# Weight loads cut into quarters, a moved product and moved softmax weights in a fused attention and MoE kernel

## The chip, the cores and the metric

One core of one Trainium2 chip. The metric is device time in microseconds (us) of one execution. Engine names are those of the profile: PE (matmul) with PEld (its weight load), DVE, ACT, POOL, SP. SP issues the large loads and does nothing else; its DMAs go to the queue called q1, hardware_dynamic. DMAs that POOL issues go to q0, software_dynamic. Both queues are served by the same 16 DMA engines.

## The reference, cut to what matters

```python
# 1. decayed linear attention over q, k, v -> x  [3072 tokens, 512]
logits = x @ phi                                   # 2. soft MoE: 8 experts, 4 slots each
d = exp(logits - logits.max(0)); d /= d.sum(0) + 1e-9
slot_input = (d.T @ x).reshape(8, 4, 512)
slot_out[e] = maximum(slot_input[e] @ w1a[e], 0) @ w2a[e]
c = exp(logits - logits.max(1)); c /= c.sum(1) + 1e-9
x2 = c @ slot_out
noisy = x2 @ w_gate + log1p(exp(x2 @ w_noise)) * noise     # 3. top-2 MoE
top2 = the two largest of noisy; top2_w = exp(top2_l - max) / (sum + 1e-9)
for e, k: out[mask] += top2_w * (maximum(x2[mask] @ w1b[e], 0) @ w2b[e])
```

w1a, w2a (moe_w1, moe_w2) are the weights of the soft MoE, w1b, w2b (moe2_w1, moe2_w2) those of the top-2 MoE. Each has 8 units, one for each expert, of 2,048 KB (2.097 MB): 128 partitions with 16 KB each.

## The kernel before

The work has four stages on one core.

- **Attention and logits** (to about 140 us): 24 tiles of 128 tokens, with chunk loads and halves of w1a on SP's queue.
- **Slots** (to about 183 us): PE multiplies the slot inputs by w1a (L794) and w2a (L814), expert after expert. `ring_used` counts the units that PE has used up; SP's later loads wait for it, since they land in the same places.
- **Passage** (183 to about 250 us): it has two strands. The *choice* strand: gate logits (L838), softplus and choice of the two experts (DVE L1404 to L1420), counts by two matmuls with a triangle and with ones (L885, L886), positions (L1424 to L1449), then a record for each (token, choice) pair (c row in two halves, weight, destinations: 35 words) which POOL writes to DRAM in one DMA of 840 KB (L560, 128 partition rows of 6,720 bytes). A sort by matmuls (L875) gives `idx`, and POOL fetches records in the new order, 128 at a time, by an indirect DMA (L574). The *SW* strand: since x2 = c @ slot_out, the kernel forms SW[e] = slot_out @ w1b[e] for each expert (`sw_product(e)`, L850; a unit of w1b by one product), takes its largest magnitude (ACT `sw_sums`, L1061), scales it and splits it into two f16 parts (`sw_high` on ACT L1065, `sw_low` on DVE L1471), spreads these over the partitions with two matmul groups for each expert (`sw_spread_parts`, L863: a "unit" is a half of an expert), and copies them back (`sw_keep`: ACT L1071 for units 0 to 7 and 12 to 15, DVE L1478 for 8 to 11).
- **Tiles** (from about 246 us): for each of 55 tiles of 128 sorted records `stage_c`, `turn_c` (L903), `hidden_b` (L922), `h_high` and `h_low`, `out_b` (L939), then POOL writes or adds rows to the output.

All order is written out by hand, by engine; each engine runs its list in order and waits on semaphores. Around the change the lists are:

- SP: w2a[2..7] (`load_w2a`), w2b[0], w1b[0..7] (`load_w1b`, L486), w2b[1] (`load_w2b`, L466, after `order_ready`), w2b[2], ... w1b[6] waits for product 2, w1b[7] for product 3 (`ring_used` 2E+3 and 2E+4).
- PE: products 0 to 4, sort (three parts, L875), product 5, product 6, spreads 0 to 3, `turn_c(0)` (needs record tile 0, staged by ACT), product 7, `hidden_b(0)`, first part of `out_b(0)`, spreads 4 to 7, `hidden_b(1)`, and the loop. A spread waits for the copy of the unit three before it, as the three banks are used in turn.
- ACT: sums of w2b[0], `sw_sums(0)`, `w2b_high(0)`, `sw_sums(1)`, Exp of the gap (L1090), `sw_sums` 2, 3, one of the sort's inputs (L1095), `sw_sums(4)`, `sw_high` 0 to 3, `sw_sums` 5, 6, keeps 0 to 3, `stage_c(0)` (L1107), keeps 4 to 7, `keep_ct(0)`, `stage_c(1)`, `sw_sums(7)`, `h_high(0)`, ..., `sw_high` 4 to 7, sums of w2b[1] (L1049), keeps 12 to 15, `h_high(1)`.
- DVE: choice, `w2b_scale_by_sum(0)`, wait for the counts, positions, destinations (L1456), the two weights of each token (L1459 to L1462), digits and comparison tables for the sort (L1495 to L1500), `idx`, `sw_low` 0 to 3, ...
- POOL: record write (L560), largest of SW[0..3], then the fetches, with the largest of SW[4..7] after the sixth.

`w2b[1]` is `w2b_in[EARLY]` in the code, since EARLY is 1; REP is 4, E is 8.

Of the kernel before, what the change touches and what calls it, by code (L numbers as in the profile page):

```python
# [9 lines left out]
ALU = mybir.AluOpType  # L10
# [5 lines left out]
def build_program(nc, chunks, phi, w1a, w2a, w_gate, w_noise, noise, w1b, w2b, consts, out, dims):  # L16
# [40 lines left out]
    with ExitStack() as ctx:  # L57
# [3 lines left out]
        def sem(name):  # L61
            return ctx.enter_context(nc.semaphore(name))
# [215 lines left out]
        w1a_last_full = sem("w1a_last_full")  # L278
        w2a_full = [sem(f"w2a_full{e}") for e in range(E)]
        w1b_full = [sem(f"w1b_full{e}") for e in range(E)]  # L280
        ring_used = sem("ring_used")
        w2b_full = [sem(f"w2b_full{e}") for e in range(E)]
        w2b_sum_ready = sem("w2b_sum_ready")
# [76 lines left out]

        SW_GROUPS = ((0, 4), (4, E))
        W2B_SUMS = 2
        sw_out = [ps[:, 2 + e // 2, e % 2 * QF:(e % 2 + 1) * QF] for e in range(E)]
        SC = ((0, 1), (2, 3))
        Y, ST, T_X, LG = range(4, 8)
# [37 lines left out]
        @block.sync  # L403
        def _(sp):
            def load_words(to, g, at, full):
                sp.dma_start(to.unsqueeze(1), chunks[bass.ds(g, 1), :, at:at + to.shape[1]]
                             .rearrange("g p m -> p g m")).then_inc(full, 16)

            def load_kv(g):
                if g >= KV_DEPTH:  # L410

                    sp.wait_ge(scores_ready, g - KV_DEPTH + 1)
                    sp.wait_ge(v_decayed, g - KV_DEPTH + 1)
                load_words(kv_in[g % KV_DEPTH], g, 0, kv_full[g % KV_DEPTH])

            def load_qk(g):
                if g >= QK_DEPTH:
                    wait_consumed(sp, (g - QK_DEPTH) // NC, (g - QK_DEPTH) % NC)
                load_words(qk_in[g % QK_DEPTH], g, 2 * DM, qk_full[g % QK_DEPTH])

            load_words(kv_in[0][:, 0:DM], 0, 0, turned_full)
            load_words(qk_in[0][:, 0:DM], 0, 2 * DM, turned_full)
            sp.dma_start(const_sb[:, 0:y_dec_at], consts[:, 0:y_dec_at]).then_inc(const_full, 16)
            load_words(kv_in[0][:, DM:2 * DM], 0, DM, kv_full[0])
            load_words(qk_in[0][:, DM:2 * DM], 0, 3 * DM, qk_full[0])
            load_kv(1)
            load_qk(1)
            sp.dma_start(const_sb[:, y_dec_at:ident_at], consts[:, y_dec_at:ident_at]).then_inc(y_dec_full, 16)
            load_qk(2)
            load_kv(2)  # L430
            sp.dma_start(phi_sb[:, :, :], phi.rearrange("(c p) s -> p c s", p=P)).then_inc(phi_full, 16)
            sp.dma_start(ident_stack[:, :], consts[:, ident_at:ident_at + P + SL]).then_inc(ident_full, 16)

            HALF = UNIT // 2

            def w1a_half(e, half, full):
                words = slice(half * HALF, (half + 1) * HALF)
                sp.dma_start(w1a_home[e][:, words], w1a[e, :, words]).then_inc(full, 16)

            ahead = 0  # L440
            for g in range(3, NT):
                load_qk(g)
                load_kv(g)
                more = (g - 2) * 2 * (E - 1) // (NT - 3)
                for half in range(ahead, more):
                    w1a_half(half // 2, half % 2, w1a_early)
                ahead = more
                if g == NC:
                    sp.dma_start(gates[:, :, 0:E], w_gate.rearrange("(c p) e -> p c e", p=P)).then_inc(small_full, 16)
                    sp.dma_start(gates[:, :, E:2 * E], w_noise.rearrange("(c p) e -> p c e", p=P)).then_inc(small_full, 16)  # L450
            assert ahead == 2 * (E - 1)

            def load_w2b(o):

                if o in (3, 6):

                    sp.wait_ge(w2b_lo_ready, {3: 2, 6: 1}[o])
                else:
                    sp.wait_ge(ring_used, {1: E + 3, 2: 2 * E + 6, 4: 2 * E + 7, 5: 2 * E + 8, 7: 2 * E + 2}[o])
                if o == EARLY:  # L460
                    sp.wait_ge(order_ready, 1)
                else:

                    sp.wait_ge(h_hi_ready, 3 * (o - EARLY) - 2)
                e = sp.value_load(order_expert[0:1, o:o + 1], min_val=0, max_val=E - 1)
                sp.dma_start(w2b_in[o].unsqueeze(1), w2b[bass.ds(e, 1), :, :]  # L466
                             .rearrange("e p m -> p e m")).then_inc(w2b_full[o], 16)

            def load_first_w2b():

                sp.wait_ge(ring_used, E + 2)
                sp.dma_start(w2b_in[0], w2b[0, :, :]).then_inc(w2b_full[0], 16)

            def load_w2a_words(e, first, last):
                words = slice(first, last)
                sp.dma_start(w2a_home[e][:, words], w2a[e, :, words]).then_inc(w2a_full[e], 16)

            def load_w2a(e):

                sp.wait_ge(ring_used, (None, None, 1, 2, 3, 5, 7, 8)[e])  # L480
                sp.dma_start(w2a_home[e], w2a[e, :, :]).then_inc(w2a_full[e], 16)

            def load_w1b(e):

                sp.wait_ge(ring_used, (E + 1, E + 6, E + 4, E + 5, E + 7, E + 8, 2 * E + 3, 2 * E + 4)[e])
                sp.dma_start(w1b_home[e], w1b[e, :, :]).then_inc(w1b_full[e], 16)  # L486

            wait_consumed(sp, B - 1, NC - 3)
            w1a_half(E - 1, 1, w1a_last_full)
            sp.wait_ge(scores_ready, NT)  # L490
            sp.wait_ge(v_decayed, NT)
            w1a_half(E - 1, 0, w1a_last_full)
            sp.dma_start(noise_t, noise[:, :, :]).then_inc(noise_full, 16)
            sp.wait_ge(x_t_ready, NT)
            load_w2a_words(0, 0, 3 * UNIT // 4)
            sp.wait_ge(slot_in_done, NG - 1)
            last_tiles = (NT - 1 - GROUPS[-1][0]) * DM
            load_w2a_words(1, last_tiles, UNIT)
            sp.wait_ge(logits_kept, NT)
            load_w2a_words(0, 3 * UNIT // 4, UNIT)  # L500
            sp.wait_ge(slot_in_done, NG)
            load_w2a_words(1, 0, last_tiles)
            for e in range(2, E):
                load_w2a(e)
            load_first_w2b()
            for e in range(E):
                load_w1b(e)
            for o in range(EARLY, E):
                load_w2b(o)
# [107 lines left out]
        def _(pe):  # L617
# [190 lines left out]
            for e in range(E):  # L808
                w = w2a_home[e].rearrange("p (c m) -> p c m", c=FC)
                pe.wait_ge(w2a_full[e], 32 if e < 2 else 16)  # L810
                for f in range(FC):
                    at = e * FC * SL + f * SL
                    for j in range(REP):
                        last = nc.tensor.matmul(bank[5][j * SL:(j + 1) * SL, 0:P], h1_blocks[:, at:at + SL],  # L814
# [27 lines left out]
            def sw_product(e):  # L842
                w = w1b_home[e].rearrange("p (c f) -> p c f", c=DC)
                if e % 2 == 1:

                    pe.wait_ge(sw_sum_ready, e)
                pe.wait_ge(w1b_full[e], 16)
                for d in range(DC):
                    for j in range(REP):
                        last = nc.tensor.matmul(sw_out[e][j * SL:(j + 1) * SL, :], slot_out_t[:, d, 0, :],  # L850
# [42 lines left out]
            for part in range(2 * NT // LO_PART):  # L893
                sort_rows(part)
            sw_product(5)
            sw_product(6)
            pe.wait_ge(sw_lo_ready, 4)
            for e in range(4):
                sw_spread_parts(e)

            def turn_c(i, r, to):
                pe.wait_ge(c_staged, i + 1)
# [85 lines left out]
        def _(act):  # L988
# [50 lines left out]
            def w2b_sum_part(e, part, unused):  # L1039
                done = W2B_SUMS * e + part  # L1040
                if part == 0:
                    act.wait_ge(w2b_full[e], 16)
                    if e < EARLY:

                        act.wait_ge(ring_used, 4)
# [38 lines left out]
            nc.scalar.activation(soft, soft, ACT.Ln, bias=1.0).then_inc(softplus_ready, 1)  # L1084
            w2b_sums(0, junk_slots[0])
            sw_sums(0)
            w2b_high(0)
            sw_sums(1)
            act.wait_ge(gap_ready, 1)
            nc.scalar.activation(wts[:, 1, :], wts[:, 0, :], ACT.Exp).then_inc(gap_exp_ready, 1)  # L1090
            sw_sums(2)
            sw_sums(3)

# [4 lines left out]
            for e in range(4):  # L1098
                sw_high(e)
            sw_sums(5)  # L1100
            sw_sums(6)
            for unit in range(4):
                sw_keep(unit)

            def stage_c(i, r, arrival):
                act.wait_ge(*arrival)
# [53 lines left out]
        def _(dve):  # L1160
# [259 lines left out]
            nc.vector.tensor_tensor(chosen, one1, one2, ALU.add).then_inc(chosen_ready, 1)  # L1420

            w2b_scale_by_sum(0)
            dve.wait_ge(ranks_done, 1)
            link(nc.vector.tensor_copy(cnt, bank[0][:, 256:256 + E * NT].rearrange("p (e t) -> p e t", e=E)))  # L1424
            link(nc.vector.memset(reset, 1.0))
# [28 lines left out]
            for n in range(2):  # L1454
                for part in range(2):
                    last = nc.vector.scalar_tensor_tensor(out=rec_src[:, n, :, SL + 1 + part], in0=late[:, (n + part) % 2, :],  # L1456
                                                          scalar=float(NOWHERE), in1=tok[:, :], op0=ALU.mult, op1=ALU.add)
            dve.wait_ge(gap_exp_ready, 1)
            link(nc.vector.tensor_scalar(wts[:, 2, :], wts[:, 1, :], 1.0, 1e-9, ALU.add, ALU.add))  # L1459
            link(nc.vector.reciprocal(wts[:, 3, :], wts[:, 2, :]))  # L1460
            nc.vector.tensor_copy(rec_src_f[:, 0, :, SL], wts[:, 3, :])
            nc.vector.tensor_tensor(rec_src_f[:, 1, :, SL], wts[:, 1, :], wts[:, 3, :], ALU.mult).then_inc(rec_ready, 1)  # L1462

            def sw_scales(group):
                first, last = SW_GROUPS[group]
# [198 lines left out]
```

## Time and profile before

| what | us |
|---|---|
| three runs | 566.98, 569.61, 570.52; median 569.61 |
| the profiled execution | 568.12 |
| its span in the trace | 566.4 |
| mean granted TensorE clock | 0.965 of full |

The profile is of one execution. The span is what the trace covers, 1.7 us less than that execution's time; times in the rows are us from the span's start.

### The profile page before, as it was taken

Reading aid. Unit: us, or ns where it says so; the run is one execution under the profiler, and the core shown is the slowest. Engines: PE = TensorE matmul, PEld = TensorE weight load, DVE = VectorE, ACT = ScalarE, POOL = GpSimd, SP = SyncE. Lnnn points to the kernel's source line nnn. Section 1 sums busy time; section 2 is a strip of 40 time slices with the busy share of each in tenths; the row PEclk is TensorE's granted clock in tenths of the full one; section 3 lists DMA queues with packets and bytes.
Section 4 is the critical chain, followed back from the end, with each engine's and each line's share of the span. In section 5 each row is a group of like instructions: output and inputs, shape, how many; then the busy total and the mean of one; then the engine's idle time right before and its main releaser. Section 6 shows DMA issues by size and latency. Waiting matters only on the chain.

```text
span 566.4 us, 13481 instructions
## 1 busy us (share of the span) xinstructions
PE 513.6 (91%) x4845; PEld 302.4 (53%) x4846; DVE 277.4 (49%) x449; ACT 187.5 (33%) x345; POOL 256.7 (45%) x216
## 2 busy tenths in 40 slices
PE   4899999997986576689999999999999999999992
PEld 4777778774466333334545454545454545454541
DVE  1766656463610589464273737373737242434240
ACT  0122221222000463664545455555552222222120
POOL 1221222121000012535577778777777766666532
PEclk9999999999798689879999999999999999999997
DMA  7899899987999999425335552222232332424310
GB/s 256 309 366 367 310 343 353 336 299 269 358 429 423 427 425 427 157 93 185 132 113 190 192 186 45 43 37 54 39 59 38 53 55 42 56 38 50 48 18 2
DMA packets 29622, 107.90 MB, mean 191 GB/s; under 512 B 11263, under 2 KB 12527, under 8 KB 24464
## 3 DMA queue, kind: packets, MB, share of 16 engines
q1 hardware_dynamic: 15408, 92.89, 42.7%
q0 software_dynamic: 14176, 14.49, 14.3%
q8 instruction: 26, 0.43, 0.3%
q14 instruction: 12, 0.10, 0.1%
HBM read 93.87 MB, written 29.43 MB: 218 GB/s over the span
## 4 chain that ended last, share of the span: by engine, by line
PE 81%; DMA 8%; issue 5%; DVE 3%; ACT 1%; POOL 1%; SPq 0%; DVEq 0%; POOLq 0%
PE ps L939 50%; PE ps L676 5%; PE ps L922 4%; PE ps L629 4%; PE ps L670 4%; DMA w_region<-moe_w 4%; PE ps L794 3%; PE ps L661 3%; PE ps L683 2%; DMA records<-rec_region 2%; PE ps L650 1%; DMA rec_region<-records,idx 1%; PE ps L643 1%; PE ps L705 1%; DMA w_region<-chunks 1%
## 5 line engine op out<-in xcount | busy, mean ns | idle before, releaser
L939 PE MATMUL ps<-w_region,s_region 128*128 (+1 forms) x1320 | 296.1, 381 | 1.1 <-ACT s_region L1118 1.1
L939 PEld LDWEIGHTS ps<-w_region,s_region 128*128 128x128 f16 x1320 | 127.3, 98 | 145.8 <-issue 5.1
L1540 DVE SCALAR_TENSOR_TENSOR s_region<-ps,s_region 128x1024 f16<-128x1024 f32 x55 | 67.3, 1224 | 149.1 <-ACT s_region L1118 143.4
L1118 ACT ACTIVATE s_region<-ps 128x1024 f16<-128x1024 f32 x55 | 56.4, 1025 | 183.0 <-PE ps L922 138.8
L580 POOL DMA_INDIRECT out<-s_region,rec_region x41 | 56.2, 1370 | 53.4 <-DVE s_region L1569 50.3
L586 POOL DMA_INDIRECT out<-s_region,rec_region x42 | 67.8, 1615 | 15.4 <-issue 12.3
L574 POOL DMA_INDIRECT rec_region<-records,idx x55 | 59.1, 1075 | 27.6 <-issue 16.4
L517 POOL TENSOR_TENSOR s_region<-w_region,s_region 128x512 f32<-128x512 f32 x22 | 23.0, 1043 | 90.1 <-PE ps L683 73.7
L922 PEld LDWEIGHTS ps<-s_region,sw_region 128*128 (+1 forms) x440 | 29.4, 98 | 15.4 <-issue 2.7
L1569 DVE TENSOR_SCALAR s_region<-ps,rec_region,y_scale 128x512 f32<-128x512 f32 x42 | 33.8, 804 | 6.8 <-PE ps L939 5.3
L922 PE MATMUL ps<-s_region,sw_region 128*128 128x128 f16 x440 | 34.1, 220 | 2.1 <-ACT sw_region L1071 2.1
L1171 DVE TENSOR_TENSOR sw_region<-ps,s_region 128x512 f32<-128x512 f32 x24 | 16.6, 692 | 34.2 <-PE ps L676 34.2
L1342 DVE SCALAR_TENSOR_TENSOR w_region<-w_region,w2b_scale 128x2048 f16<-128x2048 f32 x14 | 32.6, 2342 | 0.0
L1031 ACT ACTIVATE w_region<-w_region,w2b_scale 128x2048 f16<-128x2048 f32 x14 | 27.8, 2003 | 3.0 <-DVE w2b_scale L1336 3.0
L550 POOL PARTITION_ALL_REDUCE w2b_sum<-w2b_sum x8 | 3.2, 397 | 53.8 <-ACT w_region L1049 53.5
L580 POOL DMA_INDIRECT out<-r_region,rec_region x13 | 19.6, 1507 | 17.2 <-DVE r_region L1569 16.4
L991 ACT ACTIVATE s_region<-ps 128x128 f32<-128x128 f32 x24 | 6.7, 278 | 52.5 <-PE ps L643 52.5
L586 POOL DMA_INDIRECT out<-r_region,rec_region x13 | 20.7, 1592 | 5.0 <-issue 4.2
L1049 ACT ACTIVATE r_region<-w_region 128x2048 f16<-128x2048 f32 x12 | 23.0, 1914 | 0.0
L629 PE MATMUL ps<-w_region 64*128 64x128 f32 x192 | 15.8, 310 | 5.2 <-DMA w_region<-chunks 5.2
L1164 DVE TENSOR_TENSOR sw_region<-ps,s_region 128x512 f32<-128x512 f32 x24 | 15.4, 680 | 9.2 <-PE ps L629 9.2
L1164 DVE TENSOR_TENSOR s_region<-ps,s_region 128x512 f32<-128x512 f32 x24 | 15.4, 680 | 6.6 <-PE ps L629 6.6
(241 smaller groups left out, 572.3 us busy)
## 6 DMA issues: line engine op xcount, KB each, us to landing
w_region<-moe_w SPq DMA_DIRECT2D x18, 2048.0 KB, 16.9
w_region<-chunks SPq DMA_DIRECT2D x34, 512.0 KB, 6.7
w_region<-moe_w SPq DMA_DIRECT2D x14, 1024.0 KB, 9.0
s_region<-moe_w SPq DMA_DIRECT2D x4, 2048.0 KB, 17.4
sw_region<-chunks SPq DMA_DIRECT2D x12, 512.0 KB, 6.5
s_region<-moe_w SPq DMA_DIRECT2D x2, 1024.0 KB, 9.2
s_region<-moe_w SPq DMA_DIRECT2D x1, 1536.0 KB, 6.3
out<-s_region,rec_region POOLq DMA_INDIRECT x83
```

Of the source, the lines that this page charges most:

```text
L574: nc.gpsimd.indirect_dma_start(rec_i[:, i * RW:(i + 1) * RW], None, records[:, :], bass.IndirectOffsetOnAxis(ap=idx[:, i:i + 1], axis=0), ...
L580: nc.gpsimd.indirect_dma_start(out[:, :], bass.IndirectOffsetOnAxis(ap=rec_i[:, i * RW + SL + 1:i * RW + SL + 2], axis=0), y_sb[i % DEPTH] ...
L586: nc.gpsimd.indirect_dma_start(out[:, :], bass.IndirectOffsetOnAxis(ap=rec_i[:, i * RW + SL + 2:i * RW + SL + 3], axis=0), y_sb[i % DEPTH] ...
L629: last = nc.tensor.matmul(bank[SC[c % 2][i]][:, n * P:(n + 1) * P], kt_in[g % KV_DEPTH][rows, n, :], qt_in[g % QK_DEPTH][rows, n, :], star ...
L676: last = nc.tensor.matmul(bank[Y][h % 2 * D:(h % 2 + 1) * D, h // 2 * P:(h // 2 + 1) * P], v_dec[c % 2][:, h * D:(h + 1) * D], probs[c % 2 ...
L922: last = nc.tensor.matmul(bank[2 + 2 * r + f // 4][:, f % 4 * P:(f % 4 + 1) * P], sw_parts[:, bass.ds(e, 1), f * P:(f + 1) * P].rearrange( ...
L939: last = nc.tensor.matmul(bank[6 + r], h[:, r, f, :], w2b_parts[:, bass.ds(o, 1), part, f, :].rearrange("p e m -> p (e m)"), start=(first ...
L1118: nc.scalar.activation(h_hi[:, r, :, :].rearrange("p c t -> p (c t)").rearrange("p (a n) -> p a n", a=2), ps[:, 2 + 2 * r:4 + 2 * r, :], A ...
L1164: last = nc.vector.tensor_tensor(probs[c % 2][:, i, :, :], bank[SC[c % 2][i]][:, :].rearrange("p (n t) -> p n t", n=NP), causal[:, :].unsq ...
L1342: last = nc.vector.scalar_tensor_tensor(out=w2b_parts[:, e, 1, chunks, :], in0=w2b_in[e].rearrange("p (c m) -> p c m", c=FC)[:, chunks, :] ...
L1540: nc.vector.scalar_tensor_tensor(out=h_lo[:, r, :, :].rearrange("p c t -> p (c t)").rearrange("p (a n) -> p a n", a=2), in0=ps[:, 2 + 2 * ...
L1569: nc.vector.tensor_scalar(y_sb[r], bank[6 + u % 2], rec[:, bass.ds(i * RW + SL, 1)], y_scale[:, bass.ds(o, 1)], ALU.mult, ALU.mult).then_i ...
```

## The change

- w1b[3] to w1b[7] are loaded by four DMAs each (quarters of the columns: 4 KB of each partition for each DMA) in place of one with 16 KB of each partition; the product waits for all four. w2b[1] is loaded so as well.
- w2a[7] is loaded in two halves, and PE waits for the second half only before its fifth chunk.
- PE runs spreads 0 and 1 between products 5 and 6 (the kernel before: all four spreads after product 6). ACT's `sw_sums(6)` goes behind keeps 0 to 3.
- The four DVE instructions that make the weights (L1459 to L1462) go from the end of the record's chain to just before DVE's wait for the counts; ACT's Exp of the gap, on which they wait, goes from behind `sw_sums(1)` to ahead of `w2b_high(0)`. The destinations' last instruction now releases the record write.

```diff
--- before.py
+++ after.py
@@ -278,6 +278,7 @@
         w1a_last_full = sem("w1a_last_full")
         w2a_full = [sem(f"w2a_full{e}") for e in range(E)]
         w1b_full = [sem(f"w1b_full{e}") for e in range(E)]
+        w2a_last_full = sem("w2a_last_full")
         ring_used = sem("ring_used")
         w2b_full = [sem(f"w2b_full{e}") for e in range(E)]
         w2b_sum_ready = sem("w2b_sum_ready")
@@ -360,6 +361,7 @@
 
         SW_GROUPS = ((0, 4), (4, E))
         W2B_SUMS = 2
+        FINE = 3
         sw_out = [ps[:, 2 + e // 2, e % 2 * QF:(e % 2 + 1) * QF] for e in range(E)]
         SC = ((0, 1), (2, 3))
         Y, ST, T_X, LG = range(4, 8)
@@ -463,8 +465,11 @@
 
                     sp.wait_ge(h_hi_ready, 3 * (o - EARLY) - 2)
                 e = sp.value_load(order_expert[0:1, o:o + 1], min_val=0, max_val=E - 1)
-                sp.dma_start(w2b_in[o].unsqueeze(1), w2b[bass.ds(e, 1), :, :]
-                             .rearrange("e p m -> p e m")).then_inc(w2b_full[o], 16)
+                parts = REP if o == EARLY else 1
+                for q in range(parts):
+                    words = slice(q * UNIT // parts, (q + 1) * UNIT // parts)
+                    sp.dma_start(w2b_in[o][:, words].unsqueeze(1), w2b[bass.ds(e, 1), :, words]
+                                 .rearrange("e p m -> p e m")).then_inc(w2b_full[o], 16)
 
             def load_first_w2b():
 
@@ -478,12 +483,21 @@
             def load_w2a(e):
 
                 sp.wait_ge(ring_used, (None, None, 1, 2, 3, 5, 7, 8)[e])
-                sp.dma_start(w2a_home[e], w2a[e, :, :]).then_inc(w2a_full[e], 16)
+                if e == E - 1:
+                    sp.dma_start(w2a_home[e][:, 0:UNIT // 2], w2a[e, :, 0:UNIT // 2]).then_inc(w2a_full[e], 16)
+                    sp.dma_start(w2a_home[e][:, UNIT // 2:UNIT], w2a[e, :, UNIT // 2:UNIT]).then_inc(w2a_last_full, 16)
+                else:
+                    sp.dma_start(w2a_home[e], w2a[e, :, :]).then_inc(w2a_full[e], 16)
 
             def load_w1b(e):
 
                 sp.wait_ge(ring_used, (E + 1, E + 6, E + 4, E + 5, E + 7, E + 8, 2 * E + 3, 2 * E + 4)[e])
-                sp.dma_start(w1b_home[e], w1b[e, :, :]).then_inc(w1b_full[e], 16)
+                if e < FINE:
+                    sp.dma_start(w1b_home[e], w1b[e, :, :]).then_inc(w1b_full[e], 16)
+                else:
+                    for q in range(REP):
+                        words = slice(q * UNIT // REP, (q + 1) * UNIT // REP)
+                        sp.dma_start(w1b_home[e][:, words], w1b[e, :, words]).then_inc(w1b_full[e], 16)
 
             wait_consumed(sp, B - 1, NC - 3)
             w1a_half(E - 1, 1, w1a_last_full)
@@ -809,6 +823,8 @@
                 w = w2a_home[e].rearrange("p (c m) -> p c m", c=FC)
                 pe.wait_ge(w2a_full[e], 32 if e < 2 else 16)
                 for f in range(FC):
+                    if e == E - 1 and f == FC // 2:
+                        pe.wait_ge(w2a_last_full, 16)
                     at = e * FC * SL + f * SL
                     for j in range(REP):
                         last = nc.tensor.matmul(bank[5][j * SL:(j + 1) * SL, 0:P], h1_blocks[:, at:at + SL],
@@ -844,7 +860,7 @@
                 if e % 2 == 1:
 
                     pe.wait_ge(sw_sum_ready, e)
-                pe.wait_ge(w1b_full[e], 16)
+                pe.wait_ge(w1b_full[e], 16 if e < FINE else 16 * REP)
                 for d in range(DC):
                     for j in range(REP):
                         last = nc.tensor.matmul(sw_out[e][j * SL:(j + 1) * SL, :], slot_out_t[:, d, 0, :],
@@ -893,10 +909,12 @@
             for part in range(2 * NT // LO_PART):
                 sort_rows(part)
             sw_product(5)
+            pe.wait_ge(sw_lo_ready, 4)
+            sw_spread_parts(0)
+            sw_spread_parts(1)
             sw_product(6)
-            pe.wait_ge(sw_lo_ready, 4)
-            for e in range(4):
-                sw_spread_parts(e)
+            sw_spread_parts(2)
+            sw_spread_parts(3)
 
             def turn_c(i, r, to):
                 pe.wait_ge(c_staged, i + 1)
@@ -1039,7 +1057,7 @@
             def w2b_sum_part(e, part, unused):
                 done = W2B_SUMS * e + part
                 if part == 0:
-                    act.wait_ge(w2b_full[e], 16)
+                    act.wait_ge(w2b_full[e], 16 * REP if e == EARLY else 16)
                     if e < EARLY:
 
                         act.wait_ge(ring_used, 4)
@@ -1084,10 +1102,10 @@
             nc.scalar.activation(soft, soft, ACT.Ln, bias=1.0).then_inc(softplus_ready, 1)
             w2b_sums(0, junk_slots[0])
             sw_sums(0)
+            act.wait_ge(gap_ready, 1)
+            nc.scalar.activation(wts[:, 1, :], wts[:, 0, :], ACT.Exp).then_inc(gap_exp_ready, 1)
             w2b_high(0)
             sw_sums(1)
-            act.wait_ge(gap_ready, 1)
-            nc.scalar.activation(wts[:, 1, :], wts[:, 0, :], ACT.Exp).then_inc(gap_exp_ready, 1)
             sw_sums(2)
             sw_sums(3)
 
@@ -1098,9 +1116,9 @@
             for e in range(4):
                 sw_high(e)
             sw_sums(5)
-            sw_sums(6)
             for unit in range(4):
                 sw_keep(unit)
+            sw_sums(6)
 
             def stage_c(i, r, arrival):
                 act.wait_ge(*arrival)
@@ -1420,6 +1438,11 @@
             nc.vector.tensor_tensor(chosen, one1, one2, ALU.add).then_inc(chosen_ready, 1)
 
             w2b_scale_by_sum(0)
+            dve.wait_ge(gap_exp_ready, 1)
+            link(nc.vector.tensor_scalar(wts[:, 2, :], wts[:, 1, :], 1.0, 1e-9, ALU.add, ALU.add))
+            link(nc.vector.reciprocal(wts[:, 3, :], wts[:, 2, :]))
+            nc.vector.tensor_copy(rec_src_f[:, 0, :, SL], wts[:, 3, :])
+            nc.vector.tensor_tensor(rec_src_f[:, 1, :, SL], wts[:, 1, :], wts[:, 3, :], ALU.mult)
             dve.wait_ge(ranks_done, 1)
             link(nc.vector.tensor_copy(cnt, bank[0][:, 256:256 + E * NT].rearrange("p (e t) -> p e t", e=E)))
             link(nc.vector.memset(reset, 1.0))
@@ -1455,11 +1478,7 @@
                 for part in range(2):
                     last = nc.vector.scalar_tensor_tensor(out=rec_src[:, n, :, SL + 1 + part], in0=late[:, (n + part) % 2, :],
                                                           scalar=float(NOWHERE), in1=tok[:, :], op0=ALU.mult, op1=ALU.add)
-            dve.wait_ge(gap_exp_ready, 1)
-            link(nc.vector.tensor_scalar(wts[:, 2, :], wts[:, 1, :], 1.0, 1e-9, ALU.add, ALU.add))
-            link(nc.vector.reciprocal(wts[:, 3, :], wts[:, 2, :]))
-            nc.vector.tensor_copy(rec_src_f[:, 0, :, SL], wts[:, 3, :])
-            nc.vector.tensor_tensor(rec_src_f[:, 1, :, SL], wts[:, 1, :], wts[:, 3, :], ALU.mult).then_inc(rec_ready, 1)
+            last.then_inc(rec_ready, 1)
 
             def sw_scales(group):
                 first, last = SW_GROUPS[group]
```

## Rows read from the trace of the kernel before

**Rows 1.** Busy time by stretch: stretch, length, each engine, clock, DMA share, GB/s

```profile
175.00:200.00 25.00, 16.49 (x224) 12.53 (x219) 8.91 (x27) 7.97 (x10) 0.37 (x1) 0.70 1.01 427
...
300.00:400.00 100.00, 100.00 (x578) 49.99 (x577) 52.85 (x61) 52.61 (x76) 75.33 (x57) 1.00 0.37 98
```

**Rows 2.** Chain that ended last, 170 to 290: start, us, what

```profile
159.34 20.12 DMA w_region<-moe_w
...
208.62 12.23 DMA records<-rec_region
...
221.77 7.31 DMA rec_region<-records,idx
```

**Rows 3.** Timeline of PE: start, us, instructions, idle before and releaser

```profile
179.50 1.07 PE L814 MATMUL ps<-w_region,sw_region 128*32 128x128 f32 x28 [0.18 <-DMA w_region<-moe_w]
...
208.86 1.93 PE L850 MATMUL ps<-w_region,slot_out_t 128*32 128x256 f32 x32 [1.81 <-DMA w_region<-moe_w]
...
220.59 1.93 PE L850 MATMUL ps<-w_region,slot_out_t 128*32 128x256 f32 x32 [2.27 <-DMA w_region<-moe_w]
...
229.96 0.64 PE L863 MATMUL ps<-s_region,r_region 128*64 128x256 f16 x4 [3.98 <-ACT sw_region L1071]
...
230.75 3.00 PE L850 MATMUL ps<-w_region,slot_out_t 128*32 128x256 f32 x32
```

**Rows 4.** DMA queue's own issues by SP: start, us, line, count

```profile
177.13 30.32 SPq L486 DMA_DIRECT2D w_region<-moe_w  x6
```

**Rows 5.** DMA issues of w1b[6], of the first fetch, of a fetch at 230

```profile
w_region<-moe_w SPq DMA_DIRECT2D x1, 2048.0 KB, 16.1
...
rec_region<-records,idx POOLq DMA_INDIRECT x1, 7.3
...
rec_region<-records,idx POOLq DMA_INDIRECT x1, 3.7
```

**Rows 6.** DMA packets by queue, 214 to 216 us: packets, MB, share of 16 engines

```profile
q1 hardware_dynamic: 38, 0.62, 72.8%
q0 software_dynamic: 36, 0.24, 28.7%
```

**Rows 7.** DMA packets of all queues, 25 to 28 us

```profile
DMA packets 306, 1.25 MB, mean 416 GB/s; under 512 B 39, under 2 KB 39, under 8 KB 268
```

**Rows 8.** DMA packets of all queues, 68 to 72 us

```profile
DMA packets 264, 1.36 MB, mean 341 GB/s; under 512 B 28, under 2 KB 28, under 8 KB 169
```

**Rows 9.** Timeline of DVE

```profile
197.14 0.18 DVE L1419 TENSOR_TENSOR r_region<-r_region 128x24 f32<-128x24 f32 x1
...
199.33 0.36 DVE L1424 COPY r_region<-ps 128x192 f32<-128x192 f32 x1 [1.09 <-PE ps L886]
...
207.47 0.17 DVE L1459 TENSOR_SCALAR r_region<-r_region 128x24 f32<-128x24 f32 x1
...
208.10 0.20 DVE L1462 TENSOR_TENSOR rec_region<-r_region 128x24 f32<-128x24 f32 x1
...
216.99 0.22 DVE L1509 SCALAR_TENSOR_TENSOR idx<-ps,r_region 128x55 int32<-128x55 f32 x1
```

**Rows 10.** Timeline of ACT

```profile
0.80 1.28 ACT L991 ACT_TABLE_LOAD   x1 [0.80 <-PEq L1650]
...
203.19 1.28 ACT L1090 ACT_TABLE_LOAD   x1
204.48 0.22 ACT L1090 ACTIVATE r_region<-r_region 128x24 f32<-128x24 f32 x1
...
223.09 0.38 ACT L1061 ACTIVATE s_region<-ps 128x256 f32<-128x256 f32 x1 [4.22 <-PE ps L850]
...
237.08 1.93 ACT L1049 ACTIVATE r_region<-w_region 128x2048 f16<-128x2048 f32 x1
```

**Rows 11.** Busy time by stretch around PE's pauses of 2 us, columns as rows 1

```profile
219.00:221.00 2.00, 0.41 (x8) 0.29 (x12) 1.90 (x5) 0.00 (x0) 0.00 (x0) 1.00 1.00 421
...
243.00:245.00 2.00, 0.19 (x2) 0.17 (x2) 0.45 (x3) 0.82 (x2) 0.00 (x0) 0.55 0.13 44
```

## Prediction, made before the changed kernel was run

> **What bounds the kernel now.** I read the busy time by stretch first. From 300 to 400 us PE is busy in all of the stretch at full clock: the tiles are bound by PE, and whatever moves their start moves the end by as much [rows 1]. From 175 to 200 us the DMA engines are full at 427 GB/s while PE is busy two thirds of the time [rows 1]. So the question is what ends last in the passage. The chain of waits answers: from the end of the slots' first products PE waits for w2a (20.12 us), and then two DMAs of POOL stand in it, the record write (12.23 us from 208.62) and the first fetch (7.31 us from 221.77) [rows 2]. The write lands at 220.85, though `idx` is there at 217.21 [rows 9]: the fetch waits for the write. Record tile 0 lands at 229.1. Only then can ACT stage it and copy on, so PE stands 3.98 us before its last early spread and starts product 7 at 230.75 [rows 3]. The unit of product 7 had been there for long: w1b[6] was issued at 204.4 and landed 16.1 us later, 220.5 [rows 5], at which product 6 starts (220.59 [rows 3]); one more unit of 2.097 MB at 427 GB/s is 4.91 us, so w1b[7] landed at about 225.5. Between 225.5 and 230.75 lies what an earlier record can win at most on PE's side.
>
> Why are these DMAs slow? The write is 840 KB, 2 us of the full rate, and takes 12.23. The packets by queue say it: from 214 to 216 us there are 38 packets of q1 and 36 of q0 [rows 6], one for one. A packet of q1 (16 KB, a row of w1b) takes 0.728 x 32 / 38 = 0.61 us of an engine, one of q0 (6,720 bytes) 0.287 x 32 / 36 = 0.26. An engine has 8 rows of the record write: 8 x 0.87 = 6.9 us, the rest is time to start and to land. A fetch among 16 KB packets took 7.3 us, one at 230 with the engines nearly empty 3.7 [rows 5].
>
> The Trainium skill, DMA: Bandwidth & Descriptors, section "Queues, rings and completion order", says that an engine goes round its queues by whole packets, typically of 9 to 17 descriptors. The turn-taking agrees with the row; nine or more of these 16 KB rows in one turn does not, as the counts alternate row by row.
>
> **The quarters (w1b[3] to w1b[7], w2b[1]).** Each row becomes four packets of 4 KB. At 416 GB/s over 16 engines, the rate of a stretch with mostly 4 KB packets [rows 7], one takes 4096 / 26,000 MB/s = 0.16 us. The write's 8 turns become 8 x (0.26 + 0.16) = 3.4 us, 3.5 less; the bound on the other side is nothing less. I take 3.5, since the count of packets in rows 6 is so even: the write takes 8.7 us. The fetch lies between 3.7 (empty) and 7.3 (16 KB neighbours) [rows 5]; estimate 3.7 + 8 x 0.16 = 5.0.
>
> The price is on q1. At 416 in place of 427 GB/s a unit takes 5.04 us, 0.13 more. That is the value I take, as that stretch is nearest in packet size; the other end is 341 GB/s, a full stretch with 4 and 8 KB packets [rows 8]: 6.15 us, 1.24 more for each. By w1b[7] five units have paid (0.65 us), by w2b[1] six (0.8). The ends are 0 and 6.2, 0 and 7.4. SP's list grows by 18 issues with w2b[1]; six of the w1b units took it from 177 to 207 us, mostly waiting [rows 4], with a unit or two still queued behind, so no issue is late. POOL's queue gets nothing new. What stands behind SP's wait for `order_ready` is w2b[1] alone, as before.
>
> **The weights on DVE.** The four instructions run from 207.47 to 208.30 [rows 9], where 0.1 us overlaps the one before them: 0.73 us off the path to the write and to `idx`. Their new place has 1.09 us of idle time before 199.33 [rows 9], so they fit, if Exp is there. Exp needs the gap, ready at 197.32 [rows 9], and takes 0.22 [rows 10]; its table load of 1.28 us is the risk. The first table load of the program ran at 0.80 [rows 10], while its activation waited for PE's first logits much later; the load is not held by the wait. So I put it ahead of the gap, in ACT's idle time, and the weights between 198.3 (199.33 less the idle 1.09) and 199.1: no cost. If it is held, Exp ends at 197.32 + 1.28 + 0.22 = 198.8, the weights at 199.6, and the gain shrinks from 0.73 to 0.4. ACT's `w2b_high(0)` keeps its place, or starts 0.6 us later if the load is held; that is covered by the 1.5 us by which the Exp and its load no longer stand between `sw_sums` 1 and 2.
>
> **w2a[7] in halves.** PE waited only 0.18 us for it [rows 3], the time in which it was behind with w2a[6]. The gain is 0 to 0.18 us, all before the choice strand. I take 0.1.
>
> **The moved spreads.** They are 16 matmuls. Four took 0.64 us at their slowest [rows 3], so 2.6 us is their upper end and 1 us my value, as those four ran behind a pause. They go into PE's 2.27 us wait for w1b[6] [rows 3]; their copies go into ACT's 4.22 us of idle before `sw_sums(6)` [rows 10]. One spread unit waits for ACT's first copy, at about 219.5, and everything is done before w1b[6] lands. They cost nothing; without cover 1 to 2.6 us. They are worth something only because the record is no longer last: ACT is then done with copies 0 to 3 before product 6.
>
> **The sum.** The write starts at 208.62 - 0.73 - 0.1 = 207.8 and lands at 216.5; `idx` is there at 216.4. The fetch follows 0.93 later, as before (220.85 to 221.77), at 217.4 in place of 221.77, and lands at 222.4 (bound 224.7, still in time). Product 6 starts at 220.6 + 0.13 x 4 = 221.1, and ACT has taken its sum at 223.6; then come stage, copy 4, the last early spread and turn, an estimate of 1.7 us (in the trace before the record landed at 229.08 and product 7 began at 230.75), to 225.3. So PE waits for w1b[7] next: 225.5 + 0.65 = 226.1, 4.6 before 230.75. Product 7 took 3.00 us then, and its like with the same 32 matmuls 1.93 [rows 3]: it ran behind PE's long pause. Now its pauses are 2 us and less. One such pause left the clock at 1.00, another, behind thin work, at 0.55 [rows 11], half of full, so 1.2 of 2.4 GHz. I take the fast product: 228.0 in place of 233.75, 5.7 us earlier. Next on ACT stand the sums of w2b[1], begun at 237.08 [rows 10], now at 231.4 if the unit is there: it lands at 226.1 + 5.04 + about 0.3 for fetch packets = 231.4. A tie; I take off 0.3. Behind it everything moves alike. Gain 5.4 us (4.3 with a slow product 7): 568.12 - 5.4 = 562.7 for an execution like the profiled one. The median of the runs lies 1.49 above that one, so the forecast is 564.2.
>
> **The rivals.**
>
> *The DMAs of POOL are not shortened* (the wait is in starting and landing, not in the turns). Then the write takes 12.2 again: 207.8 to 220.0, fetch at 221.0, record at 228.3, and product 7 behind it: 0.8 us gained, 568.8. For it: the eight turns account for only 6.9 of the 12.23 us. Against: rows 6.
>
> *Slower: the quarters starve the stream.* At 341 GB/s [rows 8] w1b[7] lands at 225.5 + 6.2 = 231.7, 0.9 later than product 7 started before, and w2b[1] at 230.4 + 7.4 + 0.3 = 238.1, 1.0 after ACT wanted it: 570.6. It decides from 1.06 us a unit on, below some 350 GB/s. Against: 416 with 268 of 306 packets under 8 KB [rows 7]. The Trainium skill, same page, section "Bandwidth", speaks for this rival: transfers should be batched to 1 MiB or more. A quarter is half of that. In between, at 380 GB/s, a unit takes 5.52, w1b[7] lands at 228.6: 2.2 + 1.0 us gained, 566.4.
>
> *Product 7 alone slow, or the next one*: 565.3; the same 1.07 us once more, either way, if the clock falls or stays up elsewhere in the passage.
>
> **How the numbers follow.** Forecast with full or low clock 0.72 (its own range 562.5 to 566); middling rate 0.12; POOL's DMAs unshortened 0.10; slower 0.06. The runs before spread by 3.5 us, so the range is 561.9 to 568.3, which leaves out most of the last two cases and the tails. About 1% (5.7 us) is what a measurement of this kernel can tell from no change. Faster by over 1% means below 563.9, close under my forecast: 0.40; slower by over 1%: 0.03; within: 0.57.
>
> **What would show it.** Right: the write lands within 9 us of its start; the fetch starts near 217.4; product 7's releaser is the DMA of w1b[7], near 226; DVE's weights stand before the wait at 199.3, with no table load on the way; the tiles start 5 us earlier, PE's time there unchanged. Wrong: packets of 4 KB that take clearly over 0.16 us; a write still near 12 us; ACT waiting for w2b[1]; a granted clock of 0.5 during product 7.

## The result, and the profile after

| | median us | runs | ratio to the kernel before, 95% interval |
|---|---|---|---|
| before | 567.46 (564.40 to 570.60) | 11 | |
| changed | 563.71 (561.69 to 566.62) | 11 | 0.9922 [0.9898, 0.9947] |
| changed, sent again with the last experiments | 564.90 (561.22 to 566.09) | 12 | 0.9940 [0.9908, 0.9971] |

The change makes the kernel 0.6 to 0.8% faster: by the ratios 4.4 us in the first comparison and 3.4 in the second, by the medians 3.8 and 3.6 (the kernel before had 568.53 beside the second). Forecast were 5.4. The profiled execution took 564.99 us (span 563.3), 3.1 less than the one of the kernel before. Line numbers have moved: L814 is now L830, L832 is L848, L850 is L866, L939 is L957.

POOL's timeline in the changed kernel:

```profile
211.01 0.74 POOL L574 DMA_DIRECT2D records<-rec_region  x1 [12.48 <-DVE rec_region L1479]
...
221.53 1.14 POOL L588 DMA_INDIRECT rec_region<-records,idx  x1 [8.56 <-DVE idx L1528]
```

The DMA issue of the record write, with the us to landing:

```profile
records<-rec_region POOLq DMA_DIRECT2D x1, 840.0 KB, 8.2
```

The write takes 8.2 us in place of 12.23 [rows 2] and lands at 219.2. The first fetch is no longer released by it but by `idx`. Yet the fetch starts only 0.24 us sooner than at 221.77 [rows 2]. Why, stands 30 us ahead, in the chain that ended last:

```profile
179.69 2.78 issue
...
186.53 1.91 PE ps L848 x8
...
220.36 0.22 DVE idx L1528
...
225.77 8.94 DMA w_region<-moe_w
```

PE stands for 2.78 us in the middle of the last w2a product, waiting for nothing that the profile shows. Its granted clock is 1.00 until 182 us and 0.50 from 184 us on, and the gate logits (L848) take 1.91 us. In the profile before, the same places are 0.80 and 1.07 us, and the clock is 0.79 from 184 to 186 us. The gate product that follows starts at 189.23, before at 186.10: 3.1 us later, of which 0.8 was there at the first w2a product (161.78 against 160.97). The choice strand is late by that much: the record write starts 2.4 us later than before (3.1 less the weights' 0.7), `idx` comes 3.4 us later, and `order_ready`, SP's issue of w2b[1] and its landing follow. Whether the change does this, or this execution did, is a question for the experiments.

Product 7 on PE, which stands behind `turn_c(0)` (228.21 us), and ACT around it:

```profile
228.37 1.93 PE L866 MATMUL ps<-w_region,slot_out_t 128*32 128x256 f32 x32
```

```profile
227.02 0.31 ACT L1125 ACTIVATE s_region<-rec_region 128x128 f16<-128x128 f16 x1 [0.91 <-DMA rec_region<-records,idx]
...
234.74 1.91 ACT L1067 ACTIVATE r_region<-w_region 128x2048 f16<-128x2048 f32 x1 [0.44 <-DMA w_region<-moe_w]
```

Record tile 0 still comes last before product 7 here, 2.4 us sooner than before [rows 3], and product 7 is a fast one. ACT's sums of w2b[1] start 2.3 us sooner than at 237.08 [rows 10], and now wait for its landing.

The weights are where they were forecast, DVE first, then ACT:

```profile
201.90 0.20 DVE L1445 TENSOR_TENSOR rec_region<-r_region 128x24 f32<-128x24 f32 x1
202.46 0.36 DVE L1447 COPY r_region<-ps 128x192 f32<-128x192 f32 x1 [0.36 <-PE ps L902]
```

```profile
198.40 1.28 ACT L1106 ACT_TABLE_LOAD   x1
200.49 0.22 ACT L1106 ACTIVATE r_region<-r_region 128x24 f32<-128x24 f32 x1 [0.80 <-DVE r_region L1437]
```

The table load ran ahead of the Exp's wait, and DVE still idles 0.36 us before the counts' copy.

The turns of the queues, 215 to 217 us:

```profile
q0 software_dynamic: 82, 0.55, 65.7%
q1 hardware_dynamic: 85, 0.30, 37.5%
```

Row for row again, 82 against 85, now with 4 KB rows: 1.032 x 32 us of engine time (16 engines for 2 us) for some 83 pairs, so a turn of 0.40 us against 0.87 [rows 6]. Eight turns are 3.8 us shorter by that, and the write is 4.0 shorter.

### The profile page after: what moved, and what is told of

Its sections match the earlier page's. It is cut to its first block, busy times and chain, and to the rows that moved or that the text cites. A ratio compares the mean times of both kernels' runs of the same rounds, so it can differ in the third digit from the quotient of the medians.

```text
span 563.3 us, 13506 instructions
## 1 busy us (share of the span) xinstructions
PE 515.7 (92%) x4845; PEld 305.0 (54%) x4846; DVE 277.4 (49%) x449; ACT 187.4 (33%) x345; POOL 257.3 (46%) x216
## 4 chain that ended last, share of the span: by engine, by line
PE 82%; DVE 7%; DMA 4%; issue 3%; ACT 1%; POOL 1%; SPq 0%; DVEq 0%; POOLq 0%
PE ps L957 49%; PE ps L940 4%; PE ps L690 4%; PE ps L643 4%; PE ps L684 3%; PE ps L808 3%; PE ps L830 3%; PE ps L675 3%; PE ps L697 2%; DMA w_region<-chunks 2%; DMA w_region<-moe_w 2%; PE ps L664 1%; PE ps L657 1%; PE ps L719 1%; ACT r_region L1067 1%
## 5 line engine op out<-in xcount | busy, mean ns | idle before, releaser
L957 PE MATMUL ps<-w_region,s_region 128*128 (+1 forms) x1320 | 296.1, 381 | 1.1 <-ACT s_region L1136 1.1
L957 PEld LDWEIGHTS ps<-w_region,s_region 128*128 128x128 f16 x1320 | 127.4, 98 | 145.7 <-issue 4.2
```

What stands on the lines that cost most here:

```text
L957: last = nc.tensor.matmul(bank[6 + r], h[:, r, f, :], w2b_parts[:, bass.ds(o, 1), part, f, :].rearrange("p e m -> p (e m)"), start=(first ...
```

## Experiments

Each was run in 5 rounds (the seventh in 3) beside the kernel before. Each ratio is to the kernel before in the same rounds; its 95% interval stands in brackets.

**1. w1b whole again.**

```diff
-        FINE = 3
+        FINE = E
```

> The changed kernel with w1b[3] to w1b[7] loaded whole again (16 KB rows); w2b[1] stays in quarters, all else stays. Theory (the gain comes from the packet size beside POOL's DMAs): the record write takes about 12 us again (8.2 in the changed kernel), the first fetch starts 3 to 4 us later and lands about 6 to 7 us after its start, so product 7 starts about 4 us later and the gain over the kernel before shrinks from 4.4 to about 1 us (0.7 of it the weights): ratio 0.998. Rival (the gain comes from the weights and the reordered spreads): the ratio stays at 0.992 to 0.993.

Measured: 567.98, ratio 0.9983 [0.9948, 1.0017]. POOL's timeline and the queues' packets, 217 to 219 us:

```profile
211.13 0.74 POOL L574 DMA_DIRECT2D records<-rec_region  x1 [12.49 <-DVE rec_region L1479]
224.20 2.34 POOL L588 DMA_INDIRECT rec_region<-records,idx  x1 [11.11 <-DMA records<-rec_region]
```

```profile
q1 hardware_dynamic: 42, 0.61, 70.9%
q0 software_dynamic: 43, 0.29, 34.3%
```

The write is back at 12.2 us, the fetch at 7.84, and product 7 at 233.69, 5.3 later than in the changed kernel from nearly the same start of the write (211.13 against 211.01). The packet size carries the gain: without the quarters none of it can be told from zero.

**2. The old order of spreads.**

```diff
             sw_product(5)
-            pe.wait_ge(sw_lo_ready, 4)
-            sw_spread_parts(0)
-            sw_spread_parts(1)
             sw_product(6)
-            sw_spread_parts(2)
-            sw_spread_parts(3)
+            pe.wait_ge(sw_lo_ready, 4)
+            for e in range(4):
+                sw_spread_parts(e)
...
             sw_sums(5)
+            sw_sums(6)
             for unit in range(4):
                 sw_keep(unit)
-            sw_sums(6)
```

> The changed kernel with the old order on PE (products 5, 6, then spreads 0 to 3) and on ACT. Theory (record tile 0 is still the last thing before product 7): spreads 0 and 1 and their copies fit behind product 6 before the record lands, so 0 to 0.5 us are lost: ratio 0.992 to 0.993. Rival (the reordering is needed for the gain, because ACT's copies would otherwise end after the record): 1 to 2 us are lost, ratio 0.994 to 0.996, and the first staging on ACT no longer waits for the fetch.

Measured: 564.68, ratio 0.9931 [0.9903, 0.9959]. The interval reaches into both of the ranges named. In its trace ACT's stage does not wait for the fetch, as the rival had it (ACT comes to it later, behind `sw_sums(6)` and the copies). Product 6 waits 3.08 us for w1b[6], to 223.58, and product 7 follows the spreads at 229.24: the old order is on the path, but the time does not tell it from the new one.

**3. The old place of the weights.** The four DVE instructions and the Exp are put back where the diff of the change took them from.

> The changed kernel with the four weight instructions and the Exp at their old places. Theory (the path to idx and to the record write runs through them): 0.7 us are lost, ratio 0.9935; in the trace the time from the end of the position work to the write's start grows by 0.7. Rival (w1b[7] or w2b[1] bounds the passage, so the choice strand has slack): nothing is lost, ratio 0.992.

Measured: 565.11, ratio 0.9940 [0.9913, 0.9968]. From the end of the destinations' last instruction to the write there are 1.05 us, in the changed kernel 0.31: the 0.73 us are really off the choice strand. They are not seen in the time: 0.7 us is less than the interval's width.

**4. w2a[7] whole again.** One DMA in `load_w2a`, no second wait in the product.

> The changed kernel with w2a[7] in one DMA again. Theory (in this stage PE waits for its own instructions, not for w2a[7]): no difference, ratio 0.991 to 0.993, and the long pause inside the last w2a product, 2 to 3 us, stands in the trace as in the changed kernel. Rival A (the halves let PE run ahead into that pause, its clock then falls and the gate logits run slow): 1 to 2 us faster than the changed kernel, ratio 0.989, pause under 1 us. Rival B (the halves save what they were forecast to, 0.1 to 0.2 us): no difference that can be seen, but the wait for w2a[7] stands in the trace with 0.2 us or more.

Measured: 564.95, ratio 0.9951 [0.9926, 0.9977]. The interval shares its lower part with both of the changed kernel's and leaves out rival A's 0.989. But the pause of 2 to 3 us with no releaser is not there; PE waited for w2a[7] instead, far longer than the 0.2 us that rival B wanted at least:

```profile
177.85 3.27 PE L824 MATMUL ps<-w_region,sw_region 128*32 128x128 f32 x64 [2.75 <-DMA w_region<-moe_w]
```

So my theory that PE does not wait for w2a[7] in this stage is false where PE is early (here the first w2a product started at 158.02). Rival B, no difference in the time but a wait of 0.2 us or more, is the one that fits.

**5. w2b[1] whole again.**

```diff
-                parts = REP if o == EARLY else 1
+                parts = 1
```

> The changed kernel with w2b[1] in one DMA again, w1b[3] to w1b[7] still in quarters. Theory A (the stream of SP's loads now ends the passage, and 4 KB rows cost it 0.2 to 0.6 us a unit): w2b[1] lands 0.2 to 0.6 us earlier and ACT's sums of it start so much earlier: ratio 0.991 to 0.992, 0.992 at most. Theory B (the later fetches matter: with 16 KB rows beside them they take 7 us in place of 5 to 5.5 and ACT's stagings of tiles 1 and 2 wait for them): 0.5 to 1.5 us slower than the changed kernel, ratio 0.993 to 0.995, with a wait of ACT's stage for a fetch in the trace.

Measured: 562.75, ratio 0.9906 [0.9871, 0.9942]. No loss; a gain over the changed kernel cannot be told apart. The fetches beside 16 KB rows did not hold ACT up: its stagings show no wait for a fetch.

**6. Eighths.** w1b[3] to w1b[7] by 8 DMAs with 2 KB rows.

> The changed kernel with w1b[3] to w1b[7] by eighths (2 KB rows, 8 DMAs a unit). Turns theory (an engine alternates row by row between the queues): the record write takes 8 x (0.26 + 0.08) = 2.7 us in its turns, 0.6 less than with quarters, 7.6 us in all in place of 8.2. Stream theory: 2 KB rows cost the stream again what 4 KB rows did or more, and the passage is bound by it, so the time is 1 to 3 us longer than that of the changed kernel: ratio 0.994 to 0.997. Rival (the write and fetch bound the passage): 0.5 us faster than the changed kernel, ratio 0.991.

Measured: 566.77, ratio 0.9953 [0.9926, 0.9979]. The queues' packets, 211 to 212 us, and all packets, 206 to 208, where nothing of POOL's was under way:

```profile
q0 software_dynamic: 50, 0.34, 80.2%
q1 hardware_dynamic: 49, 0.09, 23.7%
...
DMA packets 422, 0.77 MB, mean 384 GB/s; under 512 B 47, under 2 KB 47, under 8 KB 422
```

Turns again row for row, and eight of them are 2.7 us, but the write still takes 7.8 us in all: up to 4.0 us after its issue no packet of q0 moves (in the kernel before up to 3.5 us), and no row size shortens that. The stream falls to 384 GB/s. The ratio is 0.0031 above that of the changed kernel's first comparison and 0.0013 above that of its second, 1.8 and 0.7 us, and the intervals overlap. The ratio lies in the stream theory's range, and the rival's 0.991 lies outside the interval.

**7. All of w2a[2] to w2a[7] and w1b in quarters.**

> Price of 4 KB rows alone: w2a[2] to w2a[7] and all of w1b by quarters (everything else as in the changed kernel), where from 160 to 200 us nothing of POOL runs beside the stream. By the forecast's term (416 against 427 GB/s) a window of 160 to 200 us shows 416 GB/s, and w1b[0], 8 units into the stream, lands 1 us later than else. By its other end (341 GB/s) it shows under 350 and w1b[0] lands 10 us later. Ratio to the kernel before 0.994 to 0.996 in the first case (0.13 to 0.2 us for each of 9 more units, on the bound), over 1.01 in the second.

Measured: 566.38, ratio 0.9931 [0.9899, 0.9962]. All packets, 160 to 200 us:

```profile
DMA packets 4069, 16.45 MB, mean 411 GB/s; under 512 B 451, under 2 KB 451, under 8 KB 3936
```

This is the price of 4 KB rows by itself: 411 GB/s against 427 [rows 1], 5.10 us a unit against 4.91. The Trainium skill (DMA: Bandwidth & Descriptors, "Bandwidth") says to batch DMAs to 1 MiB or more to have at least 75% of the peak. On 512 KB DMAs that stand in line that rule is not seen at work: they lose 4%. PE waited 2.04 us for w2a[7], now in quarters and awaited whole.

**8. Late quarters.** `FINE = 5`, w2b[1] whole.

> The changed kernel with quarters for w1b[5], w1b[6] and w1b[7] only; w1b[3], w1b[4] and w2b[1] whole. Theory (only the rows that are in the queue beside the record write and the first fetch need to be small, and the stream's end bounds the passage): the write still takes 8 to 9 us, w1b[4] to w1b[7] land 0.3 to 0.5 us earlier, w2b[1] 0.5 to 1 earlier: 0.5 to 1 us faster than the changed kernel, ratio 0.990 to 0.991. Rival (rows of w1b[4] are still in the queue when the write starts, and later fetches suffer from w2b[1]): the write takes 10 us or more, and the time is 1 us longer than the changed kernel's, ratio 0.994.

Measured: 564.31, ratio 0.9915 [0.9884, 0.9946]. The write took 7.8 us, so no small rows are needed before w1b[5]. The half us to be won on the stream is within the interval. Product 7 starts at 227.38 and waits 0.20 us for w1b[7], a near tie: before it ACT had waited 0.67 us for record tile 0.

**9. Quarters alone.** The kernel before with w1b[3] to w1b[7] in quarters.

> The kernel before with w1b[3] to w1b[7] in quarters and nothing else. Theory (the shorter write and fetch are nearly all of the gain): the write takes 8 us, the fetch waits for idx and not for the write, product 7 starts 3 to 4 us earlier: ratio 0.993 to 0.995. Rival (all parts must go together, because the old order of PE and the late weights hold the passage by themselves): less than 1.5 us, ratio 0.998 or more.

Measured: 563.56, ratio 0.9914 [0.9886, 0.9942]. ACT and POOL:

```profile
232.87 1.91 ACT L1059 ACTIVATE r_region<-w_region 128x2048 f16<-128x2048 f32 x1 [0.37 <-DMA w_region<-moe_w]
```

```profile
219.74 1.14 POOL L584 DMA_INDIRECT rec_region<-records,idx  x1 [8.54 <-DVE idx L1519]
```

All of the gain is there with this part alone, more than I expected of it. The fetch waits for `idx`, product 7 starts 4.1 us sooner than before, at 226.67, and ACT waits for w2b[1], whole as it is.

**10. Weights alone.** The kernel before with the weights and the Exp moved.

> The kernel before with the weights and their Exp moved and nothing else. Theory (the record write is the bound there, and its start moves with the weights): 0.7 us faster, ratio 0.999, the write 0.7 us sooner behind the position work, its length still about 12 us. Rival (the table load of 1.28 us is held by the Exp's wait and the weights come late): no gain or up to 0.4 us slower, with a late start of the counts' copy.

Measured: 567.24, ratio 0.9962 [0.9926, 0.9997], which holds 0.999 and ends just short of no change. The profiled execution was one of the two longest (571.12 us), so of its trace only lengths are used: the write took 12.60 us, as expected, and started 0.32 us behind the destinations; DVE still idled 0.36 us before the counts' copy, so the rival of late weights is out.

**11. Halves alone.** The kernel before with w2a[7] in halves.

> The kernel before with w2a[7] in halves and nothing else. Forecast's term: 0.1 us. Theory from the runs so far (relative to the landing of w1b[0], the gate logits start 6.0 us ahead with the halves and 5.0 without): the choice strand and so the record write come up to 1 us sooner, 0 to 1 us faster, ratio 0.998 to 1.000, where PE is not held by its own pauses. Rival (PE runs ahead into its instruction pause and its clock falls): the gate logits' 8 matmuls take 1.89 us in place of 1.07, and the time is the same or 1 us longer.

Measured: 568.55, ratio 0.9993 [0.9961, 1.0024]. No effect. The gate logits took 1.15 us here, and 1.89 in experiment 9 without the halves: the rival's slow product is not tied to them. From the first w2a product to the gate product's start there are 24.6 to 27.6 us in the nine profiles with halves (mean 26.5) and 25.1 to 27.1 in the four with w2a[7] whole (mean 26.2).

**12. The changed kernel again.**

> The changed kernel itself, once more, beside the three parts. Theory: ratio 0.992 to 0.993 as before, and in this profile, if the choice strand is not late, product 7 waits for w1b[7], as the forecast had it. If record tile 0 is again what releases product 7, the late choice strand is the kernel's rule and not the draw of one execution.

Measured: 564.90, ratio 0.9940 [0.9908, 0.9971]. Product 7 on PE, and the busy time of 227 to 229 us:

```profile
226.46 3.56 PE L866 MATMUL ps<-w_region,slot_out_t 128*32 128x256 f32 x32 [1.72 <-DMA w_region<-moe_w]
```

```profile
227.00:229.00 2.00, 2.00 (x27) 1.23 (x21) 0.00 (x0) 0.00 (x0) 0.00 (x0) 0.50 0.94 347
```

Here the same program shows what was forecast: with a choice strand in time, product 7 is released by w1b[7], at 226.46 (forecast 226.1). But it runs at half clock (0.50 granted), 3.56 us. The slots were no quicker in this profile: from the first w2a product to the gate product 27.4 us pass, as in the first profile (27.5). The strand is in time because that first product started at 158.11 and not at 161.78.

Product 7 in the profiles with quarters:

| kernel | starts | waits for | idle before | length |
|---|---|---|---|---|
| changed | 228.37 | record tile 0 | under 0.1 | 1.93 |
| 9, quarters alone | 226.67 | spreads | under 0.1 | 1.93 |
| 2, old spreads | 229.24 | spreads | under 0.1 | 1.93 |
| 3, old weights | 226.12 | spreads | under 0.1 | 1.93 |
| 4, w2a[7] whole | 226.98 | spreads | under 0.1 | 1.93 |
| 8, late quarters | 227.38 | w1b[7] | 0.20 | 1.93 |
| 12, changed again | 226.46 | w1b[7] | 1.72 | 3.56 |
| 5, w2b[1] whole | 229.15 | w1b[7] | 1.90 | 3.15 |
| 6, eighths | 229.31 | w1b[7] | 2.03 | 3.22 |
| 7, all in quarters | 229.34 | w1b[7] | 1.74 | 3.37 |

The end of product 7 carries the time. In all fourteen profiles, those with 16 KB rows included, 333.4 to 334.7 us pass from it to the end of the execution, while product 7 itself ends between 228.1 and 237.1.

## Why the prediction was right

**The turns** were the heart of it, and they held: forecast were 0.42 us a turn, measured 0.40, with rows of 16, 4 and 2 KB each exchanged one for one. The write was forecast at 8.7 us and took 7.8 to 8.6 in the ten profiles with small rows beside it; the first fetch was forecast at 5.0 and took 5.4 to 5.8 in the seven of them that list it alone. Experiment 1 takes this part away and loses the gain, experiment 9 has it alone and keeps it. The rival that POOL's DMAs are not shortened is gone. It was right in one thing: some 4 us of the write lie ahead of its first packet and stay.

**The price of 4 KB rows** was taken at 0.13 us a unit and is 0.19 (experiment 7). The rival of a starved stream (1.06 us a unit needed) is out even at 2 KB rows: 2.097 MB at 384 GB/s is 5.46 us, 0.55 more.

**What is late next** was forecast as w1b[7] at 226.1, then w2b[1] in a tie with ACT. Of the ten profiles in the table five show w1b[7] as product 7's releaser, four of them with a wait of 1.7 us or more and one (experiment 8) with 0.2; in experiments 2, 3, 4 and 9 product 6 waited for w1b[6], and product 7 follows from that; and ACT waits for w2b[1] by 0.2 to 1.3 us in the changed kernel and in experiments 2, 3, 4 and 9, where it landed at 232.6 to 235.3 (forecast 231.4). So SP's stream ends last in nine of ten. The changed kernel's own first profile is the exception, with its late choice strand. Experiment 12 shows that this is not the program's rule, and the times under experiment 11 show no sign of the halves in it. What makes the strand late in one execution and not in another stays open.

**The size** is 1.0 to 2.0 us short of the forecast 5.4. The term of the sum that was off is the end of product 7, forecast at 228.0 (start 226.1, fast product). In the changed kernel's two profiles it came at 230.3 and 230.0, 2.3 and 2.0 us late, and these executions took 2.3 and 1.8 us more than the 562.7 that the sum gave. But it was late in two ways:

- In the first profile the product was fast and its start was late: 228.37, behind the choice strand. The sum took that strand's time in the slots from the one trace before.
- In experiment 12 the start was right, 226.46, and the step that failed is "I take the fast product". PE's pause before product 7 was expected near 2 us, and I had two such pauses to go by, one with the clock kept and one with it lost [rows 11]. In all four profiles in which PE waited 1.7 us or more for w1b[7], product 7 took 3.15 to 3.56 us; where it followed at once, 1.93. The difference is 1.2 to 1.6 us.

With the slow product my own sum gave 4.3, beside the measured 4.4 and 3.4. Which of the two ways holds for how many of the executions without a profile is not shown, and no run held the clock up.

**The weights** were costed right (0.73 us off the strand, shown by experiment 3; covered on DVE with 0.36 us left) and, as the sum had it, are worth nothing at the end once the stream is the bound: no term of the forecast's last steps contains them. Experiments 3 and 9 see no loss clear of noise without them; in experiment 10, where they stand alone, the interval holds the 0.7 us expected and ends only just short of none. **The halves** were put at 0.1 us and show nothing alone. But the term was read from one execution in which PE was behind: in experiment 4, without them, PE waited 2.75 us for w2a[7]. **The moved spreads** were put at no cost and no loss of cover; that holds. The claim that they are worth something once the record is early is not shown: quarters alone do as well.

The runs before were forecast from a median of three, 569.61; with eleven it is 567.46. That the forecast 564.2 stands so near the measured 563.71 is luck: this offset of 2.1 us and the missing 1 to 2 us nearly cancel.

## What to carry to other kernels

When a small DMA on one queue crawls beside bulk loads on another, count the packets of each queue in a window: if they alternate one for one, each row of the small DMA waits for one row of the bulk queue. Here, with eight rows for each DMA engine, cutting the bulk rows from 16 to 4 KB cost the bulk 4% and gave the small DMA 4 of its 12 us. Cut only the loads that are in the queue at that moment. When a wait is removed, price the product behind the next wait at both clocks: here a PE that stood for 1.7 us or more before product 7 ran it at half speed in four of four profiles.

## What the runs showed that I had not expected

- From POOL's issue of the record write to its first packet about 4 us pass (3.5 to 4.5), beside rows of 16, 4 and 2 KB alike. It is half of the write's time now.
- PE's products of w2a have pauses of 0.5 to 2.8 us at fixed counts of matmuls (28, then each 128), for which the profile names no releaser. When the last of them is long, the gate logits run at half clock: they took 1.89 us behind pauses of 1.89 to 2.78 us (six profiles), and 1.07 to 1.15 behind 0.77 to 1.38 (four). It is no rule for short ones: in experiment 9, behind a wait of 1.63 us for w2a[7] and a pause of 0.75, they took 1.89 as well. In the changed kernel's two profiles the first w2a product started at 161.78 and 158.11, and from there to the gate product it took 27.5 and 27.4 us; over all the profiles that stretch spreads from 24.6 to 27.6, nearly as much as the change is worth.
- A pause of PE of 1.7 to 2.0 us was enough for half clock in four of four cases ahead of product 7. The length alone does not decide: ahead of product 6 the clock stayed whole behind 2.27 us in the kernel before [rows 3], 3.08 in experiment 2 and 1.57 in experiment 12, and fell behind 1.62 and 1.86 in experiments 3 and 4 (3.57 and 3.58 us for the product).
